# Masked attention and two MLPs on one core: the row statistics turned by one product and a DMA, and the sign bits from three fp32r products

## The chip, the core and the metric

One core of a Trainium2 chip runs the whole program. The metric is the device time in microseconds (us), the median over runs. Work is divided among the engines PE (TensorE, matrix products), DVE (VectorE), ACT (ScalarE) and POOL (GpSimd); SP issues all DMAs of the attention stage on one queue. Each engine runs its own list of instructions strictly in order, and the lists meet only at semaphores.

## The reference, cut to what matters

```python
q_bits = (einsum('bhsd,dk->bhsk', q, proj) > 0)      # 6 sign bits of each row
k_bits = (einsum('bhsd,dk->bhsk', k, proj) > 0)
mask   = q_bucket[:, :, :, None] == k_bucket[:, :, None, :]
scores = where(mask, scale * q @ k.T, -1e9)
scores = scores - max(scores); attn = exp(scores)
attn   = attn / (sum(attn) + 1e-9)
x      = attn @ v
# then two MLPs on x (1536 x 512, inner width 2048), with two activation functions
```

There are 16 heads (2 batches of 8), 768 rows of 64 elements each. The buckets must match exactly, and the whole is computed to nearly fp32: a number is split into a rounded half (`hi`, fp32r) and the remainder (`lo`), and products are made of the halves.

## The kernel before, in words

The attention stage runs head after head, h = 0 to 15, in pairs j with u = 0 or 1 (h = 2j + u). Pairs 1 to 5 are a hardware loop, the others are written out. `slot` is h mod 2: every per-head buffer exists twice. A head has six steps, c = 0 to 5. In step c PE does, in this order, `scores` of the chunk two steps on (two pairs of 384-column products: `k1` with `q1`, line 441, then `k2` with `q2`, line 446; in steps 4 and 5 these are chunks 0 and 1 of the next head), and `values` of chunk c (three pairs, line 460). The last step ends with `empty_rows` (line 468). Between them PE makes side products in `ps_a`, ordered by the table `uses_of`:

* `a` (line 411): the masked scores of a later head, two halves per chunk, of which DVE takes row maxima (line 754). Chunks 4 and 5 of head h+1 come in step 0 of head h, chunks 0 to 3 of head h+2 in steps 3 to 5.
* `bits` (line 408): `proj` times the raw q and k of head h+3 in plain fp32, in step 1. DVE compares with 0 (line 757, `bit01`), POOL makes penalties of it (`bit_rows`, line 631, `pen`), and SP copies them into the operands.
* `m`, the turn (lines 424 and 428): the statistics of head h+1 (`mcols`, made by POOL in `row_stats` from DVE's maxima) are turned from columns into rows by six products with the identity, in step 2 after `values`; a product of partial sums of v (`v_part`) goes with them.

ACT turns scores into p with `exps` (lines 551 and 555), DVE makes `p_lo` (`low`, line 782), which frees the scores buffer of the step. ACT's `stat_rows` (line 564, step 3) puts the four turned rows into `q2`, and the next head's first `k2` product in step 4 waits for them (`s_stat`).

SP's list for head h is: `load_raw` (h+4), `load_v` (h+2), for u = 0 also `store_rows` and `spread` of the previous pair's denominators, `fill_a` (h+3: two DMAs of q and k rows, then, behind the wait for `pen`, two of the bit rows, lines 308 and 309), `fill_b` (h+2: eight DMAs, lines 317 to 324, allowed when head h has ended), `turn_den` (h, line 362: the sums of head h into `den`).

DVE's `reciprocals` (lines 117 and 119) come at the end of step 2 of a u = 0 head and wait for the `turn_den` DMA of the head just ended. `split_qk` makes `hi` on ACT (line 537) and `lo` on POOL (line 618), and waits until `fill_b` of the slot's earlier head has landed.

Of the kernel before, what the change touches and what calls it, by code (L numbers as in the profile page):

```python
# [17 lines left out]
P = 128  # L18
# [21 lines left out]
STAT_END = STAT_ROW + STATS  # L40
PENALTY = float(2 ** 30)
# [13 lines left out]
def build_program(nc, qk, v, proj, w_in1, w_out1, alpha, w_in2, w_out2, a, b, consts, out):  # L55
    rden_dram = nc.dram_tensor("rden_scratch", (PAIRS, 2, S), F32, kind="Internal").ap()
    outer = ExitStack()
    with outer:
# [68 lines left out]
        with att:  # L127
# [8 lines left out]
            pj = sb("pj", [P, 4 * BITS])  # L136
            raw = [sb(f"raw{u}", [P, S]) for u in range(2)]
# [16 lines left out]
            v_sum = [sb(f"v_sum{u}", [P, P], F32R) for u in range(2)]  # L154
            row_max = [sb(f"row_max{u}", [P, 2, KC]) for u in range(2)]
# [18 lines left out]
            s_pj0 = sem("s_pj0")  # L174
            s_id = sem("s_id")
# [16 lines left out]
            s_stat = sem("s_stat")  # L192
            s_vs = sem("s_vs")
# [31 lines left out]
            def uses_of(left, u, first_head):  # L225
# [5 lines left out]
                if first_head:  # L231
# [12 lines left out]
                        ([], [("a", 2, 3)] if more else [])]  # L244

            FIRST = [("bits", 0, 0), ("bits", 1, 0)] + [("a", 0, c) for c in range(KC)] + \
                    [("m", 0, 0), ("a", 1, 0), ("a", 1, 1)]

            def a_chunks_done(g):

                return 2 * (KC + 2) if isinstance(g, int) and g == 0 else 2 * USES * g + 2 * (FIRST_USES - USES + 2)

            def bits_done(g):

                if isinstance(g, int) and g < 4:
                    return 2 * (1, 2, FIRST_USES + 2, FIRST_USES + 4)[g]
                return 2 * USES * g + 2 * (FIRST_USES - 3 * USES + 3)

            def turned(g):


                if isinstance(g, int) and g < 2:
                    return 2 * (KC + 3, FIRST_USES + 3)[g]
                left_out = max(0, g - HEADS + 3) if isinstance(g, int) else 0
                return 2 * USES * g + 2 * (FIRST_USES - USES + 4 - left_out)

            def halves_before(j, left):

                if isinstance(j, int) and j == 0:
                    return 2 * len(FIRST)  # L270
                return 2 * FIRST_USES + 4 * USES * j - 2 * (not left)
# [12 lines left out]
            def _(sp):  # L284
# [14 lines left out]
                def fill_a(u, jj):  # L299
                    g = 2 * jj + u  # L300
# [5 lines left out]
                    sp.dma_start(ka[u][0:D].bitcast(F32), hi[u][D:P].bitcast(F32)).then_inc(s_a_in[u], 16)  # L306
                    sp.wait_ge(s_pen, g + 1)
# [18 lines left out]
                def load_raw(u, jj):  # L326
                    g = 2 * jj + u

                    sp.wait_ge(s_hi, g - 1)
                    sp.wait_ge(s_lo, g - 1)  # L330
                    if isinstance(g, int):
                        sp.wait_ge(s_a_out, bits_done(g - 2))
                    else:

                        sp.wait_ge(s_a_out, 2 * USES * g - (12 * USES - bits_done(4)))
                    sp.dma_start(raw[u][:], qk[bass.ds(g, 1)].rearrange("a p s -> (a p) s")).then_inc(s_raw[u], 16)
# [26 lines left out]

                fill_a(0, 0)
# [31 lines left out]
            def _(pe):  # L396
                def use(kind, slot, jj, c, n):
# [3 lines left out]
                    elif c == 0:  # L401
                        pe.wait_ge(s_a_in[slot], 64 * (jj + 1))
                    for i in range(2):
# [3 lines left out]
                        if kind == "bits":  # L407
                            m = pe.matmul(ps_a[0:4 * BITS, i, 0:HALF], pj[:], raw[slot][:, half], start=True, stop=True)
                        else:
# [5 lines left out]
                def turn(slot, jj, n):  # L415


                    g = 2 * jj + slot
                    pe.wait_ge(s_mcols, g + 1)
                    for i in range(2):  # L420
                        pe.wait_ge(s_a_free, n + i - 1)
                        if i == 1:
                            pe.wait_ge(s_vpart, g + 1)
                            pe.matmul(ps_a[:, 1, HALF:HALF + D], cst[:, C_SEL:C_SEL + P], v_part[slot][:],
                                      start=True, stop=True)
                        for c in range(3):
                            k = STATS * (3 * i + c)
                            m = pe.matmul(ps_a[0:STAT_END, i, c * P:(c + 1) * P], mcols[slot][:, k:k + STAT_END],
                                          ident[:], start=True, stop=True)
                        m.then_inc(s_a_out, 1)  # L430

                def scores(slot, jj, c, t):
# [10 lines left out]
                    if c == 0:  # L443
                        pe.wait_ge(s_stat, g + 1)
# [51 lines left out]
                def pair(j, left):  # L496
                    final = not left
                    n = halves_before(j, left)
# [30 lines left out]
            def _(act):  # L529
# [16 lines left out]
                def exps(c, t):  # L546


                    p32 = ps_s[c % 2][:, :, 0:HALF]
                    act.wait_ge(s_score, t + 1)  # L550
                    nc.scalar.activation(p32, p32, ACT.Exp, scale=float(D) ** -0.5).then_inc(s_exp, 1)  # L551
                    act.wait_ge(s_exp, t + 1)
# [3 lines left out]

                def stat_rows(slot, jj):
# [3 lines left out]
                    act.wait_ge(s_b_in[slot], 128 * (jj + 1))  # L561
# [699 lines left out]
```

## Time and profile before

| what | value |
|---|---|
| time, median of 3 runs | 849.64 us (849.24 to 849.83) |
| the profiled execution | 849.61 us, span of its records 847.6 us |
| PE busy | 816.2 us (96%) |
| DVE, ACT, POOL busy | 575.8, 426.7, 283.7 us |
| granted TensorE clock, mean | 0.998 of 2.4 GHz |
| attention stage | to about 293.7 us of the span; the MLPs follow |

The span is divided by eye into the attention stage, where all engines work for one another, and the MLPs, where PE runs almost without a gap. The chain that the profile follows back from the end is nearly all MLP, because PE is released by nothing but itself there; it says little of the attention stage. Each engine's timeline over one head tells more.

### The profile page before, as it was taken

Reading aid. Unit: us, or ns where it says so; the run is one execution under the profiler, and the core shown is the slowest. Engines: PE = TensorE matmul, PEld = TensorE weight load, DVE = VectorE, ACT = ScalarE, POOL = GpSimd, SP = SyncE. Lnnn points to the kernel's source line nnn. Section 1 sums busy time; section 2 is a strip of 40 time slices with the busy share of each in tenths; the row PEclk is TensorE's granted clock in tenths of the full one; section 3 lists DMA queues with packets and bytes.
Section 4 is the critical chain, followed back from the end, with each engine's and each line's share of the span. In section 5 each row is a group of like instructions: output and inputs, shape, how many; then the busy total and the mean of one; then the engine's idle time right before and its main releaser. Section 6 shows DMA issues by size and latency. Waiting matters only on the chain.

```text
span 847.6 us, 11624 instructions
## 1 busy us (share of the span) xinstructions
PE 816.2 (96%) x3740; PEld 651.6 (77%) x3740; DVE 575.8 (68%) x886; ACT 426.7 (50%) x639; POOL 283.7 (33%) x365
## 2 busy tenths in 40 slices
PE   8899999999999799999999999998999999999996
PEld 5577777877778678888888888886788788887884
DVE  5578778787887455445333544359998788879885
ACT  1577768777777711112011210136676666667663
POOL 5366655636545499600000044555600000000000
PEclk9999999999999999999999999999999999999999
DMA  6465664575555243200000012122100100010001
GB/s 161 122 191 150 153 157 128 149 173 142 143 131 122 70 144 121 78 1 1 0 1 1 1 50 75 54 72 74 50 2 0 50 0 0 0 49 2 0 1 49
DMA packets 33988, 60.77 MB, mean 72 GB/s; under 512 B 10016, under 2 KB 12192, under 8 KB 33952
## 3 DMA queue, kind: packets, MB, share of 16 engines
q1 hardware_dynamic: 33952, 60.30, 25.9%
q8 instruction: 21, 0.34, 0.2%
q14 instruction: 15, 0.12, 0.0%
HBM read 29.51 MB, written 3.19 MB: 39 GB/s over the span
## 4 chain that ended last, share of the span: by engine, by line
PE 55%; DVE 6%; ACT 2%; issue 2%; DMA 1%; DVEq 0%; ACTq 0%
PE ps_h L980 28%; PE acc L998 27%; DVE work L1137 1%; DVE num L1141 1%; DVE num L1125 1%; DMA out<-stage 1%; DVE g_lo L1102 1%; DVE work L1131 1%; ACT work L1055 1%; DVE den_q L1118 1%; ACT work L1052 1%; DVE num L1121 0%; DVE x_lo L1150 0%; ACT g_hi L1032 0%; ACT work L1041 0%
## 5 line engine op out<-in xcount | busy, mean ns | idle before, releaser
L1032 ACT ACTIVATE g_hi<-num 128x512 fp32r<-128x512 f32 x96 | 60.9, 634 | 219.2 <-PE acc L998 200.7
L1108 DVE TENSOR_SCALAR num<-ps_h,alpha_sb 128x512 f32<-128x512 f32 x48 | 36.0, 751 | 135.7 <-PE ps_h L980 135.7
L754 DVE TENSOR_REDUCE row_max<-ps_a 128x1 f32<-128x384 f32 x192 | 97.9, 552 | 23.4 <-PE ps_a L411 22.5
L551 ACT ACTIVATE ps_s<-ps_s 128x768 f32<-128x768 f32 x96 | 76.7, 798 | 52.5 <-PE ps_s L446 52.0
L782 DVE TENSOR_TENSOR p_lo<-ps_s,p_hi 128x768 fp32r<-128x768 f32 x96 | 90.8, 946 | 16.6 <-ACT p_hi L555 16.6
L555 ACT ACTIVATE p_hi<-ps_s 128x768 fp32r<-128x768 f32 x96 | 78.0, 812 | 4.6
L1102 DVE TENSOR_TENSOR g_lo<-num,g_hi 128x512 fp32r<-128x512 f32 x96 | 73.6, 767 | 8.1 <-ACT g_hi L1032 1.4
L980 PE MATMUL ps_h<-x_hi,w_late_in_hi 128*128 128x512 f32 (+1 forms) x288 | 79.0, 396 | 0.0
L980 PE MATMUL ps_h<-x_hi,w_late_in_lo 128*128 128x512 f32 (+1 forms) x288 | 78.8, 396 | 0.0
L980 PE MATMUL ps_h<-x_lo,w_late_in_hi 128*128 128x512 f32 (+1 forms) x288 | 78.8, 395 | 0.0
L1040 ACT ACTIVATE den_q<-ps_h,abs_b 128x512 f32<-128x512 f32 x48 | 33.1, 690 | 84.8 <-PE ps_h L980 69.9
L980 PEld LDWEIGHTS ps_h<-x_lo,w_late_in_hi 128*128 128x128 f32 x288 | 54.1, 188 | 13.1
L980 PEld LDWEIGHTS ps_h<-x_hi,w_late_in_lo 128*128 128x128 f32 x288 | 54.1, 188 | 13.1
L441 PE MATMUL ps_s<-q,k 128*128 128x384 f32 x192 | 55.5, 370 | 8.6 <-DVE p_lo L782 7.5
L980 PEld LDWEIGHTS ps_h<-x_hi,w_late_in_hi 128*128 128x128 f32 x288 | 54.1, 188 | 12.6
L998 PE MATMUL acc<-w_late_out_hi,g_hi 128*128 128x512 f32 x144 | 56.9, 395 | 4.6 <-DVE g_lo L1102 4.6
L411 PE MATMUL ps_a<-ka,qa 76*128 76x384 f32 x192 | 55.8, 357 | 1.2 <-DVE row_max L754 0.5
L998 PE MATMUL acc<-g_hi,w_late_out_hi 128*128 128x512 f32 x144 | 56.4, 392 | 0.0
L998 PE MATMUL acc<-g_lo,w_late_out_hi 128*128 128x512 f32 x144 | 56.3, 391 | 0.0
L998 PE MATMUL acc<-w_late_out_hi,g_lo 128*128 128x512 f32 x144 | 56.3, 391 | 0.0
L998 PE MATMUL acc<-w_late_out_lo,g_hi 128*128 128x512 f32 x144 | 56.2, 390 | 0.0
L998 PE MATMUL acc<-g_hi,w_late_out_lo 128*128 128x512 f32 x144 | 56.2, 390 | 0.0
(127 smaller groups left out, 1760.8 us busy)
## 6 DMA issues: line engine op xcount, KB each, us to landing
stage<-in_w_in SPq DMA_DIRECT2D x26, 256.0 KB, 2.8
stage<-in_w_out SPq DMA_DIRECT2D x26, 256.0 KB, 3.1
raw<-in_qk SPq DMA_DIRECT2D x16, 384.0 KB, 3.1
q<-hi SPq DMA_DIRECT2D x32, 192.0 KB
k<-hi SPq DMA_DIRECT2D x32, 192.0 KB
v_raw<-in_v SPq DMA_DIRECT2D x16, 192.0 KB, 3.0
qa<-hi SPq DMA_DIRECT2D x16, 192.0 KB
ka<-hi SPq DMA_DIRECT2D x16, 192.0 KB
```

The source lines that it names most:

```text
L411: m = pe.matmul(ps_a[:, i, 0:HALF], qa[slot][0:BIT_ROW + 12, c * P:(c + 1) * P], ka[slot][0:BIT_ROW + 12, half], start=True, stop=True)
L441: pe.matmul(dst[:, i, 0:HALF], k1[slot][:, c * P:(c + 1) * P], q1[slot][:, i * HALF:(i + 1) * HALF], start=True, stop=False)
L551: nc.scalar.activation(p32, p32, ACT.Exp, scale=float(D) ** -0.5).then_inc(s_exp, 1)
L555: nc.scalar.activation(halves(p_hi[c % 3][:]), p32, ACT.Copy).then_inc(s_phi, 1)
L754: dve.tensor_reduce(row_max[slot][:, i, c:c + 1], ps_a[:, i, 0:HALF], AX.X, ALU.max).then_inc(s_a_free, 1)
L782: dve.tensor_tensor(halves(p_lo[c % 3][:]), ps_s[c % 2][:, :, 0:HALF], halves(p_hi[c % 3][:]), ALU.subtract).then_inc(s_plo, 1)
L980: m = pe.matmul(ps_h[f % 4][:], weight(w, f)[:, k * P:(k + 1) * P], x[:, bass.ds(t * NT + k * TOK, NT)], start=(i == 0 and k == 0), stop=( ...
L998: m = pe.matmul(acc[d][:], lhs, rhs, start=(f == 0 and n == 0), stop=(f == FC - 1 and n == 2))
L1032: nc.scalar.activation(g_hi[f % 2][:], num[f % 4][:], ACT.Copy).then_inc(s_ghi, 1)
L1040: nc.scalar.activation(den_q[f % 2][:], h, ACT.Abs, scale=abs_b[:, 0:1])
L1102: dve.tensor_tensor(g_lo[f % 2][:], num[f % 4][:], g_hi[f % 2][:], ALU.subtract).then_inc(s_glo, 1)
L1108: dve.tensor_scalar(num[f % 4][:], h, 0.0, alpha_sb[:, f:f + 1], ALU.min, ALU.mult).then_inc(s_step, 1)
```

## The change

Two things, and with them a new order of the lists.

1. The turn is one product with the identity (24 columns of statistics at once, except for head 0) and the `v_part` product. ACT copies the 24 turned rows of 128 into `stats`, and a DMA (`fill_stats`, on SP) brings them as four rows of 768 into `q2`. The turn moves ahead of `values` in step 2; `stat_rows` moves to ACT's step 2.
2. From head 4 on the bits are made from `hi` and `lo` with three fp32r products per half (`split`), and come at the end of step 4 in place of step 1, since they need `lo`. `hi` moves to ACT's step 3, `v_hi` to its step 4; on POOL `lo` comes ahead of `bit_rows`, and `v_lo` behind it.
3. `a` chunks of head h+2 move to steps 1, 3, 4 and 5. On SP `fill_stats` stands first, the two row DMAs of `fill_a` go ahead, the two bit DMAs stay in front of `fill_b`, `load_v` goes behind `spread`. On DVE the v sum (`sum_parts`) comes ahead of `low` of chunk 4.

```diff
                 return [([("a", 1, 4)], [("a", 1, 5)]),
-                        ([], [("bits", 3, 0)] if bits else []),
-                        ([], [("m", 1, 0)]),
                         ([], [("a", 2, 0)] if more else []),
-                        ([("a", 2, 1)] if more else [], [("a", 2, 2)] if more else []),
+                        ([("m", 1, 0)], []),
+                        ([], [("a", 2, 1)] if more else []),
+                        ([("a", 2, 2)] if more else [], [("split", 3, 0)] if bits else []),
                         ([], [("a", 2, 3)] if more else [])]
...
+                def fill_stats(slot, jj):
+                    g = 2 * jj + slot
+                    sp.wait_ge(s_turned, g)
+                    if due(g - 1):
+                        sp.wait_ge(s_head, g - 1)
+                    dst = q2[slot][STAT_ROW:STAT_END].rearrange("n (c p) -> n c p", c=KC)
+                    src = stats[slot][STAT_ROW:TURN_END]
+                    sp.dma_start(dst.bitcast(F32), src.bitcast(F32)).then_inc(s_stat, 16)
...
+                        if left or u == 0:
+                            fill_stats(1 - u, j + u)
                         if left > 1:
                             load_raw(u, j + 2)
-                        if left:
-                            load_v(u, j + 1)
+                        if left > 1 or (left == 1 and u == 0):
+                            fill_a_rows(1 - u, j + 1 + u)
...
+                        if left:
+                            load_v(u, j + 1)
                         if left > 1 or (left == 1 and u == 0):
-                            fill_a(1 - u, j + 1 + u)
+                            fill_a_bits(1 - u, j + 1 + u)
                         if left:
                             fill_b(u, j + 1)
                         turn_den(u, j, h)
...
+                        elif kind == "split":
+                            pe.matmul(ps_a[:, i, 0:HALF], pj_hi[:], hi[slot][:, half], start=True, stop=False)
+                            pe.matmul(ps_a[:, i, 0:HALF], pj_lo[:], hi[slot][:, half], start=False, stop=False)
+                            m = pe.matmul(ps_a[:, i, 0:HALF], pj_hi[:], lo[slot][:, half], start=False, stop=True)
...
+                    else:
+                        m = pe.matmul(ps_a[0:TURN_END, 0, 0:P], mcols[slot][:], ident[:], start=True, stop=True)
...
                     if c == 0:
-                        pe.wait_ge(s_stat, g + 1)
+                        pe.wait_ge(s_stat, 16 * (g + 1))
...
-                            if c == 4 and (left > 1 or (left == 1 and u == 0)):
+                            if c == 3 and (left > 1 or (left == 1 and u == 0)):
                                 split_qk(1 - u, j + 1 + u)
-                            if c == 1 and not (final and u == 1):
+                            if c == 4 and not (final and u == 1):
                                 split_v(1 - u, j + u)
-                            if c == 3 and not (final and u == 1):
+                            if c + 2 < KC or not (final and u == 1):
+                                exp32((c + 2) % KC, t + 2)
+                            if c == turn_step(j, u) and not (final and u == 1):
                                 stat_rows(1 - u, j + u)
...
+                            if c == 3 and not (final and u == 1):
+                                sum_parts(1 - u, j + u)
+                                n = n + 2
                             if c + 1 < KC or not (final and u == 1):
                                 low((c + 1) % KC, t + 1)
```

## Rows read from the trace of the kernel before

**Rows 1.** The page: the span, and PE's busy time and share.
```profile
span 847.6 us, 11624 instructions
...
PE 816.2 (96%) x3740; PEld 651.6 (77%) x3740; DVE 575.8 (68%) x886; ACT 426.7 (50%) x639; POOL 283.7 (33%) x365
```
**Rows 2.** Windows, heads 8 and 9: stretch, length, busy by engine, clock, DMA.
```profile
168.03:184.93 16.90, 16.40 (x88) 12.25 (x88) 13.98 (x25) 12.36 (x18) 8.23 (x17) 1.00 0.64 158
184.93:201.67 16.74, 16.43 (x88) 13.77 (x88) 12.91 (x23) 13.06 (x19) 10.85 (x13) 1.00 0.56 141
```
**Rows 3.** Timeline of PE in the first of these heads: start, length, line.
```profile
171.07 0.61 PE L441 MATMUL ps_s<-q,k 128*128 128x384 f32 x2 [0.20 <-DVE p_lo L782]
...
173.01 1.47 PE L408 MATMUL ps_a<-raw,pj 128*24 128x384 f32 x4
174.41 0.61 PE L441 MATMUL ps_s<-q,k 128*128 128x384 f32 x2
...
176.27 0.40 PE L428 MATMUL ps_a<-ident,mcols 128*100 128x128 f32 x3
...
176.99 0.56 PE L441 MATMUL ps_s<-q,k 128*128 128x384 f32 x2
...
184.58 0.51 PE L468 MATMUL ps_o<-q,v_sum 128*65 128x384 f32 x2
```
**Rows 4.** Timeline of SP's DMA issues over the same two heads.
```profile
168.27 0.52 SPq L317 DMA_DIRECT2D q<-hi  x1
...
173.46 0.77 SPq L324 DMA_DIRECT2D k<-pen  x1
174.49 0.55 SPq L362 DMA_DIRECT2D den<-o_sb  x1
...
185.17 0.52 SPq L317 DMA_DIRECT2D q<-hi  x1
...
191.45 0.55 SPq L362 DMA_DIRECT2D den<-o_sb  x1
192.36 0.35 SPq L336 DMA_DIRECT2D raw<-in_qk  x1
```
**Rows 5.** Timeline of SP before the first head.
```profile
20.19 0.78 SPq L308 DMA_DIRECT2D qa<-pen  x1
...
21.83 0.52 SPq L317 DMA_DIRECT2D q<-hi  x1
```
**Rows 6.** Timeline of DVE in the first of the two heads.
```profile
173.88 1.25 DVE L757 TENSOR_SCALAR bit<-ps_a,cst 24x384 f32<-24x384 f32 x2 [0.74 <-PE ps_a L408]
...
176.68 1.04 DVE L117 TENSOR_SCALAR den<-den 128x12 f32<-128x12 f32 x1 [0.69 <-DMA den<-o_sb]
```
**Rows 7.** Timeline of POOL in the same head.
```profile
176.22 1.46 POOL L631 TENSOR_TENSOR pen<-bit,cst 24x768 fp32r<-24x768 f32 x1 [1.42 <-DMA k<-pen]
180.73 1.84 POOL L618 TENSOR_TENSOR lo<-raw,hi 128x768 fp32r<-128x768 f32 x1 [3.05 <-ACT hi L537]
```
**Rows 8.** Timeline of ACT in the same head.
```profile
179.82 0.83 ACT L537 ACTIVATE hi<-raw 128x768 fp32r<-128x768 f32 x1
```
**Rows 9.** Timeline of DVE in head 14, where POOL stands still.
```profile
276.80 0.17 DVE L117 TENSOR_SCALAR den<-den 128x12 f32<-128x12 f32 x1 [1.84 <-DMA den<-o_sb]
277.01 0.23 DVE L119 RECIPROCAL rden<-den 128x12 f32<-128x12 f32 x1
277.15 0.89 DVE L782 TENSOR_TENSOR p_lo<-ps_s,p_hi 128x768 fp32r<-128x768 f32 x1
277.97 0.27 DVE L775 SCALAR_TENSOR_TENSOR v_sum<-vs_hi,cst,ps_a 128x64 fp32r<-128x64 f32 x1
```
**Rows 10.** Timeline of head 1: head 2's statistics ready on POOL, then step 4's `k2`.
```profile
56.68 0.21 POOL L651 TENSOR_TENSOR mcols<-neg_live,mcols 128x6 fp32r<-128x6 f32 x1
...
61.83 0.34 PE L446 MATMUL ps_s<-q,k 128*128 128x384 f32 x1
```
**Rows 11.** Timeline of PE in head 13: step 4's `k2`.
```profile
263.07 0.51 PE L446 MATMUL ps_s<-q,k 128*128 128x384 f32 x2
```

More of the change, by code:

```diff
@@ L40 @@
 STAT_END = STAT_ROW + STATS
+TURN_END = STAT_ROW + STATS * KC
 PENALTY = float(2 ** 30)
@@ L154, in build_program @@
             v_sum = [sb(f"v_sum{u}", [P, P], F32R) for u in range(2)]
+            stats = [sb(f"stats{u}", [P, P], F32R) for u in range(2)]
             row_max = [sb(f"row_max{u}", [P, 2, KC]) for u in range(2)]
@@ L244, in uses_of, with turn_step, use_counts @@
                         ([], [("a", 2, 3)] if more else [])]
+            def turn_step(j, u):
+                return 3 if isinstance(j, int) and j + u == 0 else 2
             FIRST = [("bits", 0, 0), ("bits", 1, 0)] + [("a", 0, c) for c in range(KC)] + \
                     [("m", 0, 0), ("a", 1, 0), ("a", 1, 1)]
+            def use_counts():
+                done, pair_start, n = {}, [], 0
+                for kind, g, c in FIRST:
+                    n += 2
+                    done[kind, g, c] = n
+                for h in range(HEADS):
+                    if h % 2 == 0:
+                        pair_start.append(n)
+                    left = min(2, PAIRS - 1 - h // 2)
+                    for before, after in uses_of(left, h % 2, h == 0):
+                        for kind, g, c in before + after:
+                            n += 2
+                            done["bits" if kind == "split" else kind, h + g, c] = n
+                return done, pair_start
@@ L257, in bits_done @@
-                return 2 * USES * g + 2 * (FIRST_USES - 3 * USES + 3)
+                return uses_done("bits", g, 0)
             def turned(g):
[L262 to L271, printed above, removed]
+                return uses_done("m", g, 0)
@@ L273, in over_pairs, with halves_before @@
+            def halves_before(j):
+                if isinstance(j, int):
+                    return PAIR_START[j]
+                return 4 * USES * j + (PAIR_START[2] - 8 * USES)
             def over_pairs(eng, body):
@@ L497, in pair @@
                     final = not left
-                    n = halves_before(j, left)
+                    n = halves_before(j)
                     for u in range(2):
@@ L579, in _ @@
                 split_v(0, 0)
-                stat_rows(0, 0)
-                exps(0, 0)
-                exps(1, 1)
+                first_stat_rows()
+                for c in range(2):
+                    exp32(c, c)
+                    exp_high(c, c)
                 split_qk(0, 1)
+                act.wait_ge(s_pj, 32)
+                act.wait_ge(s_pjclear, 1)
+                nc.scalar.activation(pj_hi[:, 0:4 * BITS], pj[:], ACT.Copy).then_inc(s_pjhi, 1)
                 def pair(j, left):
@@ L639, in row_stats @@
                     zero = cst[:, C_ZERO:C_ZERO + KC]
-                    max_hi, max_lo, none, none_too = (mcols[u][:, STAT_ROW:].rearrange("p (c n) -> p n c", n=STATS)[:, n]
-                                                      for n in range(STATS))
+                    cols = mcols[u][:, STAT_ROW:]
+                    if isinstance(g, int) and g == 0:
+                        cols = cols.rearrange("p (c n) -> p n c", n=STATS)
+                    else:
+                        cols = cols.rearrange("p (n c) -> p n c", n=STATS)
+                    max_hi, max_lo, none, none_too = (cols[:, n] for n in range(STATS))
                     nc.gpsimd.tensor_tensor(neg_max[:], zero, top[:], ALU.subtract)
@@ L714, in pair @@
                         if left > 1 or (left == 1 and u == 0):
+                            split_qk(1 - u, j + 1 + u)
+                        if left > 1 or (left == 1 and u == 0):
                             bit_rows(1 - u, j + 1 + u)
-                            split_qk(1 - u, j + 1 + u)
+                        if not (final and u == 1):
+                            split_v(1 - u, h + 1)
                         if u == 1 and not (isinstance(j, int) and j == 0):
@@ L748, in use @@
                     g = 2 * jj + slot
-                    if kind == "bits" and due(g):
+                    if kind != "a" and due(g):
                         dve.wait_ge(s_pen, g)
@@ L814, in pair @@
                                 maxima(1 - u, j + u, n)
-                            if c == 3 and not (final and u == 1):
-                                sum_parts(1 - u, j + u)
-                                n = n + 2
                             for kind, g, cc in steps[c][1]:
```

82 lines of the change are left out of this document (57 added, 25 removed).

## The prediction

> **What bounds the kernel now.** I read the page first, then windows head by head, then one timeline per engine over heads 8 and 9. PE is busy 96% of the span [rows 1], but a share is no bound: what matters is who ends each wait. A head takes 16.90 and 16.74 us [rows 2]. PE hands over a pair of 384-column fp32r products every 0.35 us (the head's last pair begins at 184.58, the next head at 184.93 [rows 2, 3]). A head has 24 score, 36 value, 12 `a` and 2 last products, 37 pairs or 12.95 us. The bits take from 173.01 to 174.41 and, by the same 0.09 us of waking as at 171.07 (0.61 against 0.52), 1.49 us, and the turn from 176.27 to 176.99, 0.72 us [rows 3]. That makes 15.2 us, and 1.6 us go in small waits such as the one for `p_lo` at 171.07 [rows 3]. DVE, ACT and POOL are busy 12.9 to 14.0, 12.4 to 13.1 and 8.2 to 10.9 us [rows 2]. So PE is the nearest bound and no chain through the others closes, because everything that SP and POOL make is made early: the eight DMAs of `fill_b` start 0.2 us after the head's end (168.27 and 185.17 [rows 4]). The reader should see that this earliness is what the change spends.
>
> **What leaves PE.** Three fp32r products per half are six at 0.175, 1.05 us against 1.49: 0.44 less. The turn keeps one of six identity products. Before, eight products took 0.72, 0.09 each; with five gone 0.28 is left, so 0.44 less. PE's own work falls by 0.9 to 14.3 us. ACT's copy at line 564 becomes 128 columns wide instead of 768; ACT is not the bound, so I count nothing. If only this counted, 12 heads would give some 11 us.
>
> **What is added: a lap through SP's queue.** The bits now come at the end of step 4, and the order of SP's list puts them in front of `fill_b`. I follow the chain from the second scores pair of step 4 (`k2`, the one that waits for the statistics):
>
> 1. PE: `k2`, `a`, three pairs of values: 5 pairs, 1.75 us.
> 2. Split: the six products end 1.2 us after they start. DVE ended the bits 0.65 after PE's last product (175.13 against 174.48 [rows 3, 6]). I take 1.95 for products and compare.
> 3. POOL's `pen`: 1.46 us [rows 7], with a hand-over of 0.08 before it (184.58 + 0.51 = 185.09 to SP's 185.17 is such a hand-over [rows 3, 4]) and 0.08 after it.
> 4. SP: the two bit DMAs to the first of `fill_b`, 21.83 - 20.19 = 1.64 us [rows 5]; 1.70 with loop registers.
> 5. SP: `fill_b` to `turn_den`, 174.49 - 168.27 = 6.22 and 191.45 - 185.17 = 6.28 us [rows 4]: 6.25.
>
> Sum, from `k2` to the issue of `turn_den`: 13.27 us. PE, after `k2`, needs 15 pairs, 5.3 us, to the head's end, while `fill_b` begins 7.0 us after `k2`. So `fill_b` no longer waits for the head's end but 1.5 us longer, and everything behind it on SP is late: `turn_den`, `fill_stats`, and the landing that lets ACT make the next `hi`.
>
> What `turn_den` leads to differs by head:
>
> * Next head odd: `fill_stats` is issued 0.9 us later (191.45 to 192.36 [rows 4], another DMA in the same place). Its landing is not in the trace. Nearest are `turn_den`, 174.49 to DVE's start at 176.68, 2.2 us [rows 4, 6], and the last bit-row DMA, 173.46 to POOL's 176.22, 2.75 us behind a full queue [rows 4, 7]. It is issued behind `turn_den`, so I take 2.2. With 0.1 for PE's waking (a pair of 0.61 against 0.52 [rows 2, 3]) it is 3.2 us to `k2`.
> * Next head even: DVE waits for `turn_den` at the end of step 2, with the v sum and `low` of chunk 4 queued behind it, and for that `low` waits step 4 of PE. 2.2 us to landing, 0.35 for sum and reciprocal as in head 14 (276.80 to 277.15), 0.25 v sum, 0.95 `low`, 0.5 the first scores pair with its waking [rows 3, 9]: 4.25 us to `k2`. The statistics have landed by then.
>
> The Trainium skill, page "DMA: Bandwidth & Descriptors", section on the anatomy of one DMA, speaks of a fixed cost of about 2.0 us per DMA, most of it the write receipt of the target. By it the odd heads' lap would be 0.2 us shorter and the total about 1 us less; no row shows this DMA.
>
> The late `fill_b` reaches ACT too: `hi` (h+3) waits for its last landing, 5.19 + 2.75 us after its start (168.27, 173.46, 176.22 [rows 4, 7]). `hi` and hand-over are 0.91 (179.82 to 180.73), `lo` 1.84 [rows 7, 8]: a split could start 10.8 us after `fill_b` does. The lap above has it at 6.25 + 3.2 + 1.75 = 11.2 in odd heads and later in even ones, so this stays hidden by 0.4 us.
>
> A pair of heads so takes 2 x 13.27 + 3.2 + 4.25 = 33.99 us. Before, `k2` of step 4 went from 61.83 in head 1 to 263.07 in head 13 [rows 10, 11], 201.24 us or 33.54 a pair. The 6 pairs now take 203.9 us: **+2.7**. From both sides: with hand-overs at nothing, a landing of 1.9 and 6.1 for `fill_b` a pair is 33.0 (-3.2 in all); with 2.75 for the landing and 0.2 more per lap it is 35.0 (+8.8).
>
> **At the ends.** In head 1 the lap does not bind yet. The statistics of head 2 are ready at 56.89 [rows 10]; behind them a hand-over (0.08), the turn (0.28), values, scores 5, values, an `a` and the first scores pair (0.35 each pair: 10 pairs) put `k2` at 60.75 against 61.83: -1.1. After head 13 one `a` less stands behind `k2`: -0.35. Head 14 gains the turn, but the same wait for `den` (276.80, then 0.35, 0.25 and 0.95 [rows 9]) holds step 4 where it is: 0. Head 0 is nearly as before: its DMA replaces a copy, and PE's saving covers it; uncovered it costs 1 us once. New clears on POOL and two small halves of `proj` lie in idle time before head 3; without cover, under 0.5 us. The MLPs are shifted, not changed. Sum of the ends: -1.4.
>
> Total: 849.61 + 2.7 - 1.4 = 850.9, say **851 us**. The profiled execution (849.61) and the median (849.64) agree, so nothing is corrected.
>
> **The rivals.**
>
> *SP's lap does not bind (faster).* If the bit rows were early enough, PE and the `den` wait would set the pace. Odd heads take 15.3 us, PE's 14.3 and 1.0 of small waits. In even heads `fill_b` starts at 0.2, `turn_den` at 6.5, `k2` comes at 6.5 + 4.25 = 10.7, the head ends at 16.1. A pair is 31.4, 2.1 less, 13 in all: 835. It is decided by whether steps 2 to 4 together take under 3.8 us, where I count 5.3; against it is that each is one in-order instruction with a row. Half of it, from a lap 0.5 us shorter, gives 845.
>
> *DVE's `den` operation is held by POOL (slower).* The same operation took 1.04 us at 176.68, ending at 177.72 just behind POOL's 177.68, and 0.17 us where POOL was idle [rows 6, 7, 9]. In even heads now POOL's `lo` would start about 0.4 us after `den`; if it comes first, `den` is held for up to its length. Bound by these rows at 0.87 us for six heads: 856; with a longer POOL operation (twice that) 861. The Trainium skill, "VectorE: DVE Perf Modes", section on two Vector instructions with no wait between them, says that what such an operation reads through the second SBUF read interface is shared with GpSimd. By it the rival holds whenever POOL runs, and the trace agrees in the one pair of rows.
>
> *Everything hides, and nothing is seen.* If the lap comes out at 33.5 to 33.8 a pair, the time is 848 to 850. That is inside my uncertainty, not another mechanism.
>
> **How the numbers follow.** The lap that binds as computed: 0.68 (its own range 847 to 855). `den` held: 0.14. Lap not binding or half: 0.14. A cause outside these: 0.04. The range of 8 in 10 takes in the unknown landing, half of the faster rival and the first size of the slower one: 845 to 857. Under 0.2% (1.7 us, about what a measurement can tell here) counts as no change, 847.9 to 851.3. Of the 0.68 about 0.10 is below, 0.30 within, 0.28 above. With the others: faster 0.23, same 0.31, slower 0.46.
>
> **What the profile would show.** Right: `fill_b` starts right behind the second bit DMA of line 309, 1.5 us past the head's end; PE waits in front of the second scores pair of step 4 for a DMA into `q` in odd heads by about 1 us; in even heads DVE idles 2 us or more before line 117, and PE waits for `p_lo` or for the row maxima's buffer; heads of about 16.5 and 17.5 us in turn. Wrong: heads all alike at 15.5 to 16, `fill_b` starting 0.2 us past the head's end, or the statistics' DMA landing in 1.5 us or over 3. The step that I trust least is the 6.25 + 1.70 us of SP issues, which count twelve times, and after it the landing of 2.2.

## The result, and the profile after

The changed kernel takes **852.11 us** (median of 17 runs, 850.07 to 854.79), the kernel before 849.64 (17 runs, 848.92 to 850.51). The ratio is 1.0033, 95% interval 1.0025 to 1.0041: 0.3% slower. The forecast was 851.0 with a range of 845 to 857. The runs also spread more than before, 4.7 us instead of 1.6.

The page of the kernel after, its span and PE's row, against [rows 1]:

```profile
span 850.4 us, 11539 instructions
...
PE 808.7 (95%) x3689; PEld 655.6 (77%) x3689; DVE 571.3 (67%) x887; ACT 418.7 (49%) x640; POOL 281.9 (33%) x367
```

PE has 7.5 us less to do and the span is 2.8 us longer. PE was given less work and stands still for longer. The windows of heads 8 and 9, against [rows 2], show how:

```profile
171.09:188.54 17.45, 15.84 (x84) 12.62 (x84) 13.08 (x25) 11.88 (x18) 8.50 (x15) 1.00 0.52 133
188.54:205.01 16.47, 15.77 (x85) 14.13 (x85) 12.88 (x23) 12.49 (x19) 10.52 (x16) 1.00 0.63 165
```

Heads were alike (16.90, 16.74) and now alternate: the odd head gained 0.27 us, the even one lost 0.55. PE is idle for 1.6 us in the even head, where it was for 0.5. Timelines of heads 7 and 8 of the kernel after show why, against [rows 3, 4, 6]. SP:

```profile
156.58 0.53 SPq L351 DMA_DIRECT2D q<-hi  x1
...
162.77 0.56 SPq L393 DMA_DIRECT2D den<-o_sb  x1
163.43 0.67 SPq L403 DMA_DIRECT2D q<-stats  x1
...
171.15 0.80 SPq L342 DMA_DIRECT2D qa<-pen  x1
172.00 0.76 SPq L343 DMA_DIRECT2D ka<-pen  x1
172.86 0.52 SPq L351 DMA_DIRECT2D q<-hi  x1
...
178.96 0.56 SPq L393 DMA_DIRECT2D den<-o_sb  x1
```

PE (line 506 is `k2`, lines 458 to 460 the split, 463 an `a` product):

```profile
165.57 0.62 PE L506 MATMUL ps_s<-q,k 128*128 128x384 f32 x2 [0.35 <-DMA q<-stats]
...
167.46 0.44 PE L458 MATMUL ps_a<-hi,pj_hi 128*128 128x384 f32 x1
...
168.63 0.51 PE L501 MATMUL ps_s<-q,k 128*128 128x384 f32 x2
...
181.53 0.82 PE L463 MATMUL ps_a<-ka,qa 76*128 76x384 f32 x2 [0.87 <-DVEq L856]
182.78 0.62 PE L501 MATMUL ps_s<-q,k 128*128 128x384 f32 x2 [0.43 <-DVE p_lo L864]
183.24 0.51 PE L506 MATMUL ps_s<-q,k 128*128 128x384 f32 x2
```

POOL's `lo` and `pen`, and DVE's `den`:

```profile
165.50 1.83 POOL L692 TENSOR_TENSOR lo<-raw,hi 128x768 fp32r<-128x768 f32 x1 [1.24 <-ACT hi L597]
169.66 1.46 POOL L705 TENSOR_TENSOR pen<-bit,cst 24x768 fp32r<-24x768 f32 x1 [2.33 <-DMA ka<-hi]
```
```profile
181.14 0.17 DVE L118 TENSOR_SCALAR den<-den 128x12 f32<-128x12 f32 x1 [2.92 <-DMA den<-o_sb]
```

Read it as a lap: `k2` at 165.57, split at 167.46, `pen` at 169.66, SP's bit DMAs at 171.15, `fill_b` at 172.86, `turn_den` at 178.96, its landing in DVE at 181.14, and `k2` of the even head at 183.24. `fill_b` starts 1.8 us after the head's end (171.09) and stands right behind the second bit DMA. DVE then has nothing to do for 2.92 us. PE waits first for the half of `ps_a` that DVE's v sum frees (0.87; line 856 is its semaphore, and the v sum stands behind `den` in DVE's list), then for `p_lo` (0.43).

The odd head has a second tight place. PE starts the split at 167.46, 0.13 us after POOL's `lo` ended (165.50 + 1.83). Experiment 4 shows the same 0.13 us where PE is recorded as waiting for `lo`. So `lo` arrives in odd heads just when PE wants it: in heads 3 to 11 the distance was 0.13 to 0.22 us, in even heads 1.4 to 2.8.

In the sums of the waits from 50 to 290 us, DVE's wait for `den` has grown from 5.9 to 19.7 us. The odd heads' wait of PE for the statistics is small:

```profile
DVE den L118 <- DMA den<-o_sb: 19.7, 7, 3.1
...
PE ps_a L463 <- DVEq L856: 4.9, 5, 1.1
...
PE ps_s L506 <- DMA q<-stats: 2.2, 6, 0.5
```

**Head 1.** It gained nothing, though the lap does not bind there yet. The timelines of POOL and PE, against [rows 10]:

```profile
51.33 0.62 POOL L734 TENSOR_SCALAR w_early_in_hi<-stage 128x512 fp32r<-128x512 f32 x1 [3.86 <-DMA stage<-in_w_out]
```
```profile
58.02 0.32 PE L479 MATMUL ps_a<-ident,mcols 128*120 128x128 f32 x1 [0.96 <-POOL mcols L729]
...
61.98 0.52 PE L506 MATMUL ps_s<-q,k 128*128 128x384 f32 x2
```

SP issues the staging of the weights at 44.75 (43.50 before), now behind the statistics' DMA and two DMAs of rows. POOL splits the weights 1.1 us later and `mcols` comes 1.1 us later. PE, whose turn now stands ahead of the values, waits 0.96 us for it.

**Head 4** took 19.15 us where its even neighbours took 17.4 to 17.6. Timeline of PE, then a window (the third number from the end is the granted clock):

```profile
112.12 0.82 PE L463 MATMUL ps_a<-ka,qa 76*128 76x384 f32 x2 [1.08 <-DVEq L856]
...
114.92 0.84 PE L520 MATMUL ps_o<-p_hi,v_hi 128*65 128x384 f32 x2
115.56 0.84 PE L520 MATMUL ps_o<-p_hi,v_lo 128*65 128x384 f32 x2
```
```profile
112.00:118.00 6.00, 5.45 (x20) 4.46 (x21) 4.28 (x9) 3.55 (x6) 1.82 (x1) 0.72 0.45 135
```

After the wait of 1.08 us for DVE (and 0.43 more) pairs follow each other by 0.64 us instead of 0.35, for some 3 us, and the granted clock of the window is 0.72. The dip cost this head about 1.6 us. It did not follow from the wait alone: heads 6 and 10 had a wait of 1.06 us in the same place, kept the full clock and took 17.6 us.

### The profile page after: what moved, and what is told of

The parts are those of the page before. It is cut to its first block, busy times and chain, and to the rows that moved or that the text cites. A ratio compares the mean times of both kernels' runs of the same rounds, so it can differ in the third digit from the quotient of the medians.

```text
span 850.4 us, 11539 instructions
## 1 busy us (share of the span) xinstructions
PE 808.7 (95%) x3689; PEld 655.6 (77%) x3689; DVE 571.3 (67%) x887; ACT 418.7 (49%) x640; POOL 281.9 (33%) x367
## 4 chain that ended last, share of the span: by engine, by line
PE 54%; DVE 6%; issue 2%; ACT 2%; DMA 1%; DVEq 0%; ACTq 0%
PE ps_h L1064 28%; PE acc L1082 26%; DVE work L1221 1%; DVE work L1215 1%; DVE num L1209 1%; DVE num L1225 1%; DVE g_lo L1186 1%; DVE den_q L1202 1%; DMA out<-stage 1%; ACT work L1139 1%; ACT work L1136 0%; DVE num L1205 0%; DVE x_lo L1234 0%; ACT work L1125 0%; ACT g_hi L1116 0%
## 5 line engine op out<-in xcount | busy, mean ns | idle before, releaser
L501 PE MATMUL ps_s<-q,k 128*128 128x384 f32 x192 | 53.3, 358 | 10.3 <-DVE p_lo L864 9.8
L1082 PE MATMUL acc<-g_hi,w_late_out_lo 128*128 128x512 f32 x144 | 56.2, 390 | 0.0
L1082 PE MATMUL acc<-w_late_out_lo,g_hi 128*128 128x512 f32 x144 | 56.2, 390 | 0.0
```

The costliest lines, as they stand in the source:

```text
L501: pe.matmul(dst[:, i, 0:HALF], k1[slot][:, c * P:(c + 1) * P], q1[slot][:, i * HALF:(i + 1) * HALF], start=True, stop=False)
L1082: m = pe.matmul(acc[d][:], lhs, rhs, start=(f == 0 and n == 0), stop=(f == FC - 1 and n == 2))
```

## The experiments

Each was timed against the kernel before on the same chip. The chips differ from experiment to experiment (the kernel before took 848.2 to 849.8 us on them), so compare by the ratios, which are to the kernel before, with 95% intervals. Heads are counted from the last pair of one to the last pair of the next.

**1. The bits in step 1, from the raw input.** Everything else of the change stays; the three products are not used.

```diff
-                        ([], [("a", 2, 0)] if more else []),
+                        ([], ([("a", 2, 0)] if more else []) + ([("bits", 3, 0)] if bits else [])),
...
-                        ([("a", 2, 2)] if more else [], [("split", 3, 0)] if bits else []),
+                        ([("a", 2, 2)] if more else [], []),
```

> The changed kernel with one part undone: the bits come again from one plain fp32 product of the raw rows, at the end of step 1; the turn by one product and a DMA stays, and so do all other moves. Theory (the lap through SP's queue): the penalties are early again, fill_b starts 0.2 us after the head's end, DVE's den operation is fed in time, and PE's own work (15.2 less 0.44 for the turn) sets the pace with 0.9 to 1.3 us of small waits: heads of 15.7 to 16.0 us, all alike, 12 of them 9 to 13 us less than before: 838 us, range 835 to 842. Rival (the DMA of the statistics is what costs, about 2.1 us from issue to landing where a copy took 0.8): 849 or more, with PE waiting for that DMA in step 4.

Measured: 854.43 us, ratio 1.0070 (1.0049 to 1.0092), so a miss of 16 us. The lap's waits were gone: outside head 14, where it stood before the change too, DVE waited for `den` once, for 0.22 us, and PE never for the statistics. But from head 4 on heads took 17.1 to 17.4 us, all alike. PE's timeline of this run:

```profile
161.03 1.47 PE L458 MATMUL ps_a<-raw,pj 128*24 128x384 f32 x4 [0.47 <-DVE row_max L838]
```

Two side products in a row need both halves of `ps_a`, which DVE frees one after the other, so PE waits 0.47 us at the bits, the scores behind them are late, and ACT idles 2.8 us for them. The run shows that the lap's waits need the late bits. It doesn't give their price, since its own order costs as much. A run with early bits and without that cost was not made.

**2 and 3. One useless DMA in front of `fill_b`,** in the kernel after and in the kernel before. It copies 64 rows of 512 bytes that nothing reads.

```diff
+                    sp.dma_start(extra[u][:], cst[0:D, 0:P]).then_inc(s_b_in[u], 16)
...
-                        pe.wait_ge(s_b_in[slot], 128 * (jj + 1))
+                        pe.wait_ge(s_b_in[slot], 144 * (jj + 1))
```

> The changed kernel with one useless DMA (64 rows of 512 bytes, constants to a scratch tile, about 0.6 us of issue) in front of the eight of fill_b. Theory (SP's issues lie on the lap): each of 12 laps grows by the issue, 0.6 us: +7 us on the changed kernel, 858 to 861. Rival (the time is lost elsewhere, SP has slack): no change, 851 to 853.

> The kernel before with the same useless DMA in front of fill_b. Theory (before the change SP's queue lies beside the path): nothing or nearly nothing, 849.5 to 851. Rival (SP was on the path already): +7 us, 856 or more.

After: 866.06 us, ratio 1.0204 (1.0171 to 1.0238), above the expected 858 to 861. Odd heads went from 16.45 to 17.05 and even ones from 17.5 to 18.2, so each lap is longer by about 0.65 us; on SP the useless DMA takes 0.57 us from its start to that of the next. That is 8 us in 12 laps. Of the rest, most is clock: heads 4, 6 and 10 took 19.7 to 19.8 us at a granted clock of 0.91, 1.6 us more than their even neighbours, where the kernel after has one such head. Head 0 was 1.3 us longer, head 14 0.7.

Before: 854.59 us, ratio 1.0067 (1.0047 to 1.0087), against an expectation of 849.5 to 851. Odd heads stayed at 16.75 but even ones went from 16.87 to 17.5. So in the kernel before SP had no time to spare in even heads: DVE's wait for `den` already set them.

**4. The kernel after with `den` on ScalarE's queue.** ACT issues the DMA right after its evacuation of the head (only head 15 keeps SP's).

```diff
+                    act.wait_ge(s_evac, h + 1)
+                    if due(j):
+                        act.wait_ge(s_rden, j)
+                    src = o_sb[u][DEN[u]:DEN[u] + 1, bass.ds((j % 2) * S, S)]
+                    act.dma_start(den[:, u], src.rearrange("o (p c) -> o p c", c=KC)).then_inc(s_den[u], 16)
```

> The changed kernel with the DMA of the row sums (turn_den) issued from ACT's queue, right behind the copy that it reads, in place of the end of SP's list; only the last head's stays on SP. Theory (in even heads DVE waits for that DMA and PE for DVE): the wait of about 3 us before line 118 goes, even heads fall from 17.5 to about 16.4 us, SP's lap is 0.7 us shorter, and what is left is the lap over hi and lo (16.3 us): 12 heads give 8 us, 844 us, range 841 to 847. Rival (the statistics' DMA alone holds PE, den is beside the path): 850 to 852.

Measured: **846.56 us** (6 runs), ratio 0.9964 (0.9946 to 0.9983), faster than both kernels. Windows of heads 8 and 9 of this run:

```profile
167.53:183.94 16.41, 15.86 (x84) 12.55 (x84) 13.26 (x25) 11.89 (x18) 8.55 (x15) 1.00 0.55 139
183.94:200.29 16.35, 15.65 (x85) 14.09 (x85) 13.05 (x23) 12.58 (x19) 10.50 (x16) 1.00 0.66 170
```

The even head has lost its 1.0 us. The odd head has hardly moved (16.47 to 16.35), so it is set by something that `den` doesn't touch. Timelines of SP, ACT, POOL and PE of this run close a second lap:

```profile
153.04 0.53 SPq L351 DMA_DIRECT2D q<-hi  x1
...
158.28 0.77 SPq L358 DMA_DIRECT2D k<-pen  x1
...
169.31 0.70 SPq L351 DMA_DIRECT2D q<-hi  x1
```
```profile
160.95 0.84 ACT L598 ACTIVATE hi<-raw 128x768 fp32r<-128x768 f32 x1 [1.87 <-DMA k<-pen]
```
```profile
161.96 1.84 POOL L700 TENSOR_TENSOR lo<-raw,hi 128x768 fp32r<-128x768 f32 x1 [1.12 <-ACT hi L598]
166.11 1.46 POOL L713 TENSOR_TENSOR pen<-bit,cst 24x768 fp32r<-24x768 f32 x1 [2.31 <-DVE bit L847]
```
```profile
163.93 0.43 PE L459 MATMUL ps_a<-hi,pj_hi 128*128 128x384 f32 x1 [0.49 <-POOL lo L700]
```

`fill_b` at 153.04, its last issue 5.24 later, landing and `hi` 2.67, `lo` 1.01, the split 1.97, `pen` 2.18, the two bit DMAs and the next `fill_b` 3.20: 16.27 us. That is the lap through `hi` and `lo`. The change closed it by making the bits out of `hi` and `lo`. From `fill_b` to the split it has 10.89 us here. The odd head of the kernel after has 10.88 (156.58 to 167.46), so the same lap holds there already; only the even heads wait longer for `den`.

**5. The kernel before with `den` on ScalarE's queue,** with the same edit.

> The kernel before with turn_den issued from ACT's queue, nothing else. Theory: in the kernel before even heads (16.9 us) stood just at the edge of the den wait, PE at 16.75: 1 us in all, 848.5 us, range 847.5 to 849.5. Rival (the den wait had hidden several tenths a head): 846 or less.

Measured: 849.06 us (11 runs), ratio 0.9992 (0.9983 to 1.0001): no difference to be told. Even heads fell to 16.72 us, as the odd ones, which agrees with experiment 3: 0.13 us in each of some six heads is under 1 us. So the 3 us of experiment 4 do not come from moving `den` as such.

**6 and 7. The one-product turn alone,** on the kernel before (bits from `raw` as before), without and with `den` on ACT. ACT copies the turned rows in step 2, between the exponential and the rounding of step 4, as in the kernel after, and SP issues the statistics behind the loads.

```diff
-                            if c == 3 and not (final and u == 1):
+                            if c + 2 < KC or not (final and u == 1):
+                                exp32((c + 2) % KC, t + 2)
+                            if c == turn_step(j, u) and not (final and u == 1):
                                 stat_rows(1 - u, j + u)
...
-                                exps((c + 2) % KC, t + 2)
+                                exp_high((c + 2) % KC, t + 2)
```

> The kernel before with the first part of the change alone: the turn is one product (still behind values in step 2), ACT copies the rows in its step 2, and a DMA behind load_v brings them into q2. The bits stay plain and early, and nothing else moves. Theory (the turn by DMA is worth its 0.44 us of PE; the change loses by the late bits and the den wait): odd heads 16.75 - 0.44 = 16.3 us, even heads stay at 16.9 because the same wait for the den DMA sets their step 4, which the extra DMA in the kernel before has shown: 846.5 us, range 844.5 to 848.5. Rival (the statistics' DMA costs more than the copy it replaces): 851 or more, with PE waiting for it.

> The kernel of the run before this one, and turn_den issued from ACT's queue behind the copy that it reads. Theory: the den wait goes from the even heads too, all heads 16.3 us: 843.5 us, range 841 to 846. Rival (even heads are bound by PE's small waits, not by den): as the run before, 846 to 847.

Measured: 856.66 us, ratio 1.0084 (1.0071 to 1.0097), and 856.26, ratio 1.0071 (1.0058 to 1.0084): a miss by 10 us and more. Heads took 17.12 us in both, so `den` had no part. Timelines of ACT, DVE and PE of the first:

```profile
166.39 0.27 ACT L598 ACTIVATE stats<-ps_a 24x128 fp32r<-24x128 f32 x1 [0.61 <-PE ps_a L449]
166.69 0.23 ACT L600 ACTIVATE vs_hi<-ps_a 128x64 fp32r<-128x64 f32 x1
166.81 0.81 ACT L582 ACTIVATE p_hi<-ps_s 128x768 fp32r<-128x768 f32 x1
```
```profile
167.64 0.96 DVE L823 TENSOR_TENSOR p_lo<-ps_s,p_hi 128x768 fp32r<-128x768 f32 x1 [2.10 <-ACT p_hi L582]
168.52 0.27 DVE L816 SCALAR_TENSOR_TENSOR v_sum<-vs_hi,cst,ps_a 128x64 fp32r<-128x64 f32 x1
```
```profile
168.84 0.44 PE L429 MATMUL ps_a<-ka,qa 76*128 76x384 f32 x1 [0.60 <-DVE v_sum L816]
```

ACT, in order, waits 0.61 us for the turn with the rounding behind it; DVE waits 2.10 for that, and PE 0.60 for DVE, in each head. In head 0 PE also waited 2.8 us for the late statistics' DMA, and the 6 us after it ran at a granted clock of 0.50; that head ended 4.7 us late.

**8 and 9. The turn alone once more, in the order of the kernel before.** ACT copies in step 3 ahead of the exponentials, SP issues the statistics first in the head. The second has `den` on ACT as well.

```diff
+                        if left or u == 0:
+                            fill_stats(1 - u, j + u)
                         if left > 1:
                             load_raw(u, j + 2)
...
                             if c == 3 and not (final and u == 1):
                                 stat_rows(1 - u, j + u)
```

> The kernel before with the one-product turn and its DMA alone, a second time: the turn stays where the kernel before has it (behind the values of step 2), ScalarE copies the turned rows in step 3 ahead of that step's exponentials as before, and SP issues the statistics' DMA as the first thing of a head. Theory A (the earlier version with the turn alone lost 7 us by its order: the copies stood ahead of the rounding of step 4, and SP's late issue in head 0 cost PE 2.8 us and a stretch at half clock; the turn itself is worth about 0.4 us of PE per head): head 0 ends near 50, heads are 16.3 to 16.8 with the even ones held a little by den as before, 844 to 848 us. Rival B (the turn with a DMA costs by itself, since its copy and landing end later than the direct copy): 851 us or more, with waits of PE on the DMA into q in every head.

> The same as the run with the turn alone, ahead of the exponentials, but the DMA of den is issued from ScalarE's queue. Theory A: even and odd heads alike, 16.3 to 16.4 us each, 842 to 845 us. Rival B (copy and landing of the statistics bound the heads): no faster than the run without this, 851 us or more.

Measured: 851.22 us (12 runs), ratio 1.0022 (1.0012 to 1.0033), and 850.33 (10 runs), ratio 1.0007 (0.9998 to 1.0016). The order was worth 5.4 us, as theory A said, and head 0 ended 1.0 us late instead of 4.7. But both times lie above their ranges: heads took 16.9 us, not 16.3 to 16.8, and `den` made no difference to them. PE's timeline of the first run:

```profile
147.48 0.44 PE L429 MATMUL ps_a<-ka,qa 76*128 76x384 f32 x1 [0.40 <-DVE v_sum L815]
...
161.56 0.22 PE L445 MATMUL ps_a<-ident,mcols 128*120 128x128 f32 x1
...
161.81 0.59 PE L467 MATMUL ps_s<-q,k 128*128 128x384 f32 x2
...
164.88 0.61 PE L472 MATMUL ps_s<-q,k 128*128 128x384 f32 x2 [0.37 <-DMA q<-stats]
```

The turn takes 0.25 us, so PE does save the forecast 0.44. It is handed back in waits: 0.37 for the statistics' DMA and 0.40 for the v sum, which the kernel before doesn't have, and longer ones for `p_lo` (8.5 us in sum from 50 to 290 us, against 4.4). Both theories were half right.

**10. The new bits alone.** The kernel after with the six-product turn, ACT copying the rows straight into `q2`, and no statistics' DMA.

```diff
-                        if left or u == 0:
-                            fill_stats(1 - u, j + u)
...
-                    nc.scalar.activation(stats[slot][STAT_ROW:TURN_END], ps_a[STAT_ROW:TURN_END, 0, 0:P],
-                                         ACT.Copy).then_inc(s_turned, 1)
+                    nc.scalar.activation(halves(q2[slot][STAT_ROW:STAT_END]), ps_a[STAT_ROW:STAT_END, :, 0:HALF],
+                                         ACT.Copy).then_inc(s_stat, 1)
```

> The changed kernel with the turn as before: six products, and ACT copies the four rows into q2 directly, in its step 2; no DMA of statistics. The split and all moved orders stay. Theory (two laps run through SP's queue, one over den in even heads at 17.5 us, and one over the landing of fill_b, hi, lo and the split at 16.3 us in odd ones, which the statistics' DMA only equals): heads of 16.3 to 16.4 and 17.5 us as in the changed kernel, 850 to 853 us. Rival (the statistics' DMA is the bound of the odd heads): odd heads at 15.8, 847 us or less.

Measured: 851.66 us (12 runs), ratio 1.0024 (1.0013 to 1.0035). Its steady heads, from 5 on, are those of the kernel after, 16.4 to 16.5 and 17.5 to 17.6 us in turn. So the one-product turn with its DMA neither makes nor saves anything in the steady heads of the whole change. The statistics' DMA is gone here and the odd heads are as long as with it: they are set by the lap through `hi` and `lo`, not by that DMA.

Two early heads do differ. The profiled execution took 857.17 us, the longest of the 12, and head 2 alone 21.83. PE's turn in head 1, and DVE's `den` in head 2:

```profile
56.44 0.45 PE L468 MATMUL ps_a<-ident,mcols 128*100 128x128 f32 x3
```
```profile
77.95 1.62 DVE L118 TENSOR_SCALAR den<-den 128x12 f32<-128x12 f32 x1 [4.16 <-DMA den<-o_sb]
```

In head 1 PE does not wait for `mcols`, and the head took 16.28 us. In head 2 `den` came just behind the start of POOL's `lo` (77.74 to 79.54) and ended when that did. PE waited 1.92 us for what stands behind it, and some 3 us at half pace followed.

**11. The new bits alone, `den` on ACT,** with the edits of experiments 10 and 4.

> The kernel with the new sign bits alone (six-product turn, ScalarE copies the rows straight into q2, no statistics DMA), and with den issued from ScalarE's queue. Theory A (the sign bits give the 0.35 us a head and the one-product turn nothing, since PE's other waits take it): heads 16.3 to 16.5 us, odd and even alike, 845 to 848 us, as far below the kernel before as the whole change with den from ScalarE (846.0 to 846.6). Rival B (the turn carries half of the gain): heads 16.7 to 16.8, 849 to 851 us.

Measured: **845.54 us** (6 runs), ratio 0.9961 (0.9947 to 0.9975). Windows of heads 8 and 9 and PE's split in this run:

```profile
167.21:183.61 16.40, 15.98 (x89) 12.97 (x89) 13.36 (x25) 12.42 (x18) 8.55 (x15) 1.00 0.56 135
183.61:200.09 16.48, 16.12 (x90) 14.43 (x90) 13.08 (x23) 13.15 (x19) 10.51 (x16) 1.00 0.66 171
```
```profile
180.01 0.43 PE L447 MATMUL ps_a<-hi,pj_hi 128*128 128x384 f32 x1 [0.19 <-POOL lo L674]
```

PE has five more products a head than in experiment 4, and the heads are as long. PE starts the split 0.13 us after the end of `lo` in both, from head 4 to head 11: the second lap sets 16.4 us whatever PE saves. Theory A holds: the gain is the new bits', and none of it the turn's.

**12. The kernel after, `den` on ACT, weights staged earlier.**

```diff
+                        if isinstance(j, int) and j == 0:
+                            stage_early(u)
                         if left > 1 or (left == 1 and u == 0):
                             fill_a_rows(1 - u, j + 1 + u)
-                        if isinstance(j, int) and j == 0:
-                            stage_early(u)
```

> The kernel after with den issued from ScalarE's queue, and with the two weight-staging DMAs of heads 0 and 1 ahead of the two row DMAs into qa and ka. Theory (the staging that went later by 1.2 us made GpSimd's weight pieces and so mcols of head 1 later by 1.1 us, and PE waited for it): the first scores of head 1 are fed about 1 us earlier than in the run with den alone, head 1 is 16.7 to 17.0 us rather than 17.75, and the time is 845 to 846 against 846.6. Rival (the later rows into qa and ka take it back, since the first sign product of the next head is fed by them): no difference to the run with den alone, 846 to 847.

Measured: 846.01 us (5 runs), ratio 0.9954 (0.9941 to 0.9967), not to be told from experiments 4 and 11. Head 1 took 16.65 us instead of 17.75, and PE waited 0.42 us for `mcols` instead of 0.98. Experiments 10 and 11 agree: without the statistics' DMA ahead of it the staging was issued at 43.8, `mcols` was ready at 56.2 (56.89 before), and head 1 took 16.3 us. So the late staging is the cause there. What stays open is why POOL could start on the staged weights 4.6 us after the second issue in one run and 6.6 in another. PE's timeline, heads 1 and 2:

```profile
57.77 0.32 PE L480 MATMUL ps_a<-ident,mcols 128*120 128x128 f32 x1 [0.42 <-POOL mcols L737]
...
74.86 0.31 PE L480 MATMUL ps_a<-ident,mcols 128*120 128x128 f32 x1 [1.04 <-POOL mcols L737]
...
75.30 0.88 PE L521 MATMUL ps_o<-p_hi,v_hi 128*65 128x384 f32 x2
```

The wait for `mcols` in head 2 is no work of this edit: the kernel after has it too (1.05 us), and so have experiments 4, 10 and 11. Only here did half pace follow it (pairs of 0.88 and 0.84), and head 2 took 18.67 us. In this one profile the gain of head 1 was so lost again; what the shift is worth over many executions isn't settled.

## Why the prediction was right, and where it was not

The forecast of 851.0 was 1.1 us off the median. The mechanism that it named, a lap through SP's queue with heads of about 16.5 and 17.5 us in turn, is there. In the even heads it is the one forecast. In the odd heads the length was right, but a path that the forecast took for hidden holds them too, and they are as long without the one that it named. That the total came so near is partly luck. Its steps:

* **The lap through SP's queue: right.** From `k2` to `turn_den` it was 13.39 us against 13.27. The parts, measured against forecast: `k2` to the split 1.89 (1.75), split to `pen` 2.20 (2.03), `pen` to the bit DMA 1.49 (1.54), the bit DMAs 1.71 (1.70, of which 0.06 was added to the row without a row of its own), `fill_b` to `turn_den` 6.10 (6.25). Experiment 2 confirms it: one more issue on SP is one more issue per head.
* **Next head even, 4.25 us: measured 4.28** (178.96 to 183.24). Experiment 4 confirms that `den` sets these heads.
* **Next head odd, 3.2 us: measured 2.80.** The statistics' issue comes 0.66 us behind `turn_den`, not 0.9, and `k2` 2.14 later, with PE's waking in it, not 2.3. PE's wait was 0.35 us, where about 1 was forecast. The Trainium skill, "DMA: Bandwidth & Descriptors", section on the anatomy of one DMA, has about 2.0 us of fixed cost, for DMAs that GpSimd issues. This DMA's 2.14 and `turn_den`'s 2.18, both issued by SP, lie beside it.
* **The `hi` and `lo` path hidden by 0.4 us: its length was right, that it is hidden was wrong.** The forecast had the split possible 10.8 us after `fill_b` and wanted at 11.2. With the odd step at 2.80 instead of 3.2 it was wanted at 10.9, and nothing was left to hide in. Experiment 10 decides it: without the statistics' DMA odd heads stay at 16.4 to 16.5 us. The forecast also followed the path only to the split. From there to the next `fill_b` it is 5.4 us more, and the whole is a lap of 16.3 us, the floor once `den` is out of the way.
* **The pair: 33.99 us forecast, 33.92 measured** in heads 8 and 9. In the odd head two paths end together, and only one was counted on.
* **The rival of a lap that does not bind: did not come.** It asked for under 3.8 us from the split to `fill_b`; that took 5.40. Experiment 2 made the bits early, but its own order cost as much, so the rival's 835 stays untested. Taking `den` off SP did not reach its heads of 15.3 and 16.1 us: they took 16.4.
* **No chain closes before the change: wrong for even heads.** Experiment 3 shows that `den` already set them, and experiment 5 that it cost 0.1 us a head.
* **`den` held by POOL: did not come in the kernel after.** The operation took 0.17 us in every even head there, because it starts when POOL stands still (181.14; `lo` starts at 181.78, 0.6 us later). Before, it took 0.98 to 1.25 us in six of seven. The mechanism is real: in head 2 of experiment 10 `lo` came first, and `den` took 1.62 us. The Trainium skill, "VectorE: DVE Perf Modes", section on two Vector instructions with no wait between them, says that the second SBUF read interface is shared with GpSimd; these rows agree.
* **Head 1, -1.1 us: failed.** `k2` came at 61.98, +0.15. The step took `mcols` from before, at 56.89, and did not count what its own rule asks for: the weight staging was moved behind other DMAs in SP's list, and POOL does the weights ahead of the statistics. Experiment 12 shows it, and experiment 10 shows the step with the staging early: `k2` at 60.88, where 60.75 was forecast.
* **The sum.** By the profiled spans: head 1 +0.15 (forecast -1.1), twelve laps from 61.98 to 267.01, that is 205.03 against 201.24, +3.8 (+2.7), the rest of the span -1.14 (-0.35 and nothing): +2.8 against +1.3. The laps' surplus is the clock dip of head 4, 1.6 us, which no term had; without it they are 0.5 us shorter than forecast. In the rest, the -0.35 behind head 13 did not come: PE waits 0.76 us for `p_lo` there instead of 0.21, and up to the last pair of head 15 it is +0.1. The other -1.2 lies in the MLPs, where nothing was forecast. Over the profiles of all 14 kernels this stretch takes 552.5 to 555.5 us, so it can't be put down to the change. The misses partly cancel.

What PE was to save was nearly there: the split takes 1.17 us to the next product's start (167.46 to 168.63; 1.07 in the even head), against 1.40 for the bits before [rows 3] and 1.05 forecast.

## What to carry to other kernels

When work is moved later in a period, follow the chain behind it round to where it started: two laps closed here, one over `den` that makes even heads 17.5 us and one over `hi` and `lo` of 16.3 that holds the odd ones, both longer than the 15.8 us that PE is busy in a head. A path that is hidden by a few tenths in a forecast counts as a bound until a run without its rival says otherwise. Count the issue time of a queue as work of its own, and ask whether a transfer that only has to be small and early can go from another engine's queue: moving the one of `den` was worth about 6 us in the changed kernel (from a ratio of 1.0033 to 0.9964) and nothing that could be told in the old one. An edit that takes time from an engine gives nothing if a lap elsewhere sets the pace; a run with only that edit tells so (experiments 10 and 11).

## What the runs showed of the hardware

* **Waits of 0.7 us and more of TensorE can cost its clock, and do not always.** After 0.73 and 0.42 us (head 4 of experiment 10), 1.08 and 0.43 (head 4 of the kernel after), 1.04 (experiment 12) and 2.8 (experiment 6) pairs of products came every 0.64 us instead of 0.35, the pace of the lower of the two levels (1.2 against 2.4 GHz), for 3 to 6 us. After 1.06 us in heads 6 and 10 of the kernel after, and after 1.67 in head 8 of experiment 2, they kept the full pace. All 14 kernels have the same wait of 1.51 or 1.52 us in head 0. In the profile of each, half pace came with it in 8 and not in 6. Windows of the kernel before (full clock) and of experiment 5 (0.60):

```profile
29.40:35.70 6.30, 5.49 (x28) 4.28 (x28) 4.77 (x10) 3.73 (x6) 0.00 (x0) 1.00 0.42 126
```
```profile
29.40:35.70 6.30, 6.25 (x22) 5.49 (x23) 3.26 (x6) 2.55 (x4) 0.00 (x0) 0.60 0.43 126
```

  That the wider spread of the kernel after comes from such dips was not shown. The mean granted clocks of its 17 runs, 0.990 to 0.996, go with the times only loosely: the fastest run had 0.994, one of 854.12 us 0.995.
* **A small DVE operation that starts while POOL is in one ends only with it.** The 128x12 operation on `den` takes 0.15 to 0.17 us when POOL stands still. Begun inside a POOL operation it took 0.98 to 1.25 us in the kernel before and 1.62 in experiment 10, and ended 0.03 to 0.04 us behind POOL's each time.
* **A DMA of 64 rows of 512 bytes holds SP's queue about as long as one of 64 whole rows:** 0.52 us in experiments 2 and 3, beside 0.52 to 0.61 for the rows of `hi`, six times as many bytes.
